# One wait moved on VectorE and two drains taken out of GpSimd's queue, in the expert stage of a three-stage kernel

## The reference

```python
def _moe2_ref(x, w_gate, w1, w2):            # N, D, E, F = 3072, 512, 8, 1024
    logits = x @ w_gate
    expert_idx = np.argmax(logits, axis=1)
    probs = np.exp(logits - logits.max(-1, keepdims=True))
    probs /= probs.sum(-1, keepdims=True) + 1e-09
    gate_w = probs[np.arange(N), expert_idx]
    for e in range(E):
        mask = expert_idx == e
        h = np.maximum(x[mask] @ w1[e], 0.0)
        out[mask] = gate_w[mask, None] * (h @ w2[e])
```

## Time and profile before

| | |
|---|---|
| median of 3 runs | 1037.83 us (1036.77, 1037.83, 1040.45) |
| the profiled execution's own time | 1036.77 us |
| its span | 1035.1 us |
| mean granted TensorE clock | 0.993 |
| busy: PE, DVE, ACT, POOL | 1003.8, 647.5, 583.5, 410.9 us |

### The profile page before, as it was taken

One profiled execution on the slowest core, in us unless ns is written; L12 is line 12 of the kernel. 1 busy time (PEld: TensorE's weight loads), 2 busy tenths in 40 slices (PEclk: granted clock), 3 DMA queues, 4 the chain that ended last, 5 costly groups with the idle time before them and its releaser, 6 DMA issues.

```text
span 1035.1 us, 19854 instructions
## 1 busy us (share of the span) xinstructions
PE 1003.8 (97%) x6222; PEld 819.4 (79%) x6223; DVE 647.5 (63%) x1207; ACT 583.5 (56%) x1255; POOL 410.9 (40%) x397
## 2 busy tenths in 40 slices
PE   8988999999999999999999999997999999999998
PEld 5777778888888888888888778786888888888886
DVE  5876788878867877887688679855223424325221
ACT  7877778766676667667666667624223324225221
POOL 3676444444543454455345357722111111112111
PEclk9999999999999999999999999998999999999999
DMA  8999614700920290064009942117311512411111
GB/s 301 357 403 348 256 41 135 232 1 11 314 84 0 100 307 0 10 234 163 0 18 373 366 149 72 41 42 294 123 41 48 190 42 84 159 41 40 31 48 37
DMA packets 58528, 143.26 MB, mean 138 GB/s; under 512 B 4967, under 2 KB 10727, under 8 KB 58480
## 3 DMA queue, kind: packets, MB, share of 16 engines
q1 hardware_dynamic: 51680, 121.07, 33.0%
q0 software_dynamic: 6800, 21.56, 6.2%
HBM read 71.08 MB, written 72.32 MB: 139 GB/s over the span
## 4 chain that ended last, share of the span: by engine, by line
PE 76%; issue 7%; SPq 5%; ACT 4%; DMA 3%; DVE 3%; POOL 1%; ACTq 0%; DVEq 0%; POOLq 0%
PE PS L511 20%; PE PS L670 19%; PE PS L542 14%; PE PS L551 13%; SPq L463 4%; PE PS L535 2%; ACT prob L819 2%; PE PS L613 2%; PE PS L690 2%; DMA x_raw<-w_exp 1%; PE PS L528 1%; DVE PS L1001 1%; DMA qk<-qk_all 1%; PE PS L583 1%; DMA e_raw<-w_exp 1%
## 5 line engine op out<-in xcount | busy, mean ns | idle before, releaser
L511 PE MATMUL PS<-xs,weights 128*128 (+1 forms) x1152 | 282.7, 394 | 0.0
L511 PEld LDWEIGHTS PS<-xs,weights 128*128 128x128 f32 x1152 | 212.6, 188 | 43.1
L670 PE MATMUL PS<-weights,g_hi 128*128 128x512 f32 x768 | 238.6, 392 | 7.6 <-POOL g_lo L1344 4.6
L1344 POOL TENSOR_TENSOR g_lo<-g_sb,g_hi 128x512 fp32r<-128x512 f32 x96 | 123.9, 1291 | 272.8 <-ACT g_hi L899 272.8
L670 PEld LDWEIGHTS PS<-weights,g_hi 128*128 128x128 f32 x768 | 142.8, 188 | 43.2 <-POOL g_lo L1344 9.1
L670 PE MATMUL PS<-weights,g_lo 128*128 128x512 f32 x384 | 149.6, 390 | 0.0
L542 PE MATMUL PS<-weights,xg_hi 128*128 (+1 forms) x448 | 143.3, 401 | 0.5 <-issue 0.2
L880 ACT ACTIVATE b_ln<-PS,cf 128x512 f32<-128x512 f32 x96 | 65.9, 686 | 132.8 <-PE PS L511 132.8
L551 PE MATMUL PS<-weights,h_hi 128*128 (+1 forms) x432 | 136.1, 396 | 0.1
L1347 POOL TENSOR_TENSOR den<-den,b_r 128x512 f32<-128x512 f32 x96 | 127.7, 1330 | 2.1 <-ACT b_r L907 2.1
L1099 DVE SCALAR_TENSOR_TENSOR den<-den,b_r 128x512 f32<-128x512 f32 x96 | 70.2, 731 | 50.9 <-POOL den L1347 50.9
(11 more groups left out here) (190 smaller groups left out, 1605.0 us busy)
## 6 DMA issues: line engine op xcount, KB each, us to landing
rows_by_expert<-pad_rows SPq DMA_DIRECT2D x40, 1028.0 KB, 15.1
e_raw<-w_exp SPq DMA_DIRECT2D x34, 512.0 KB, 6.7
qk<-qk_all SPq DMA_DIRECT2D x32, 480.0 KB, 6.6
vw<-v_all SPq DMA_DIRECT2D x32, 384.0 KB, 6.0
rows_by_expert<-pad_rows SPq DMA_DIRECT2D x8, 1285.0 KB, 18.2
w_raw<-w_mlp SPq DMA_DIRECT2D x16, 512.0 KB, 8.4
pad_rows<-rows_by_expert POOLq DMA_DIRECT2D x30, 257.0 KB
x_raw<-attention_out_t SPq DMA_DIRECT2D x10, 512.0 KB, 4.5
```

The costliest lines, as they stand in the source:

```text
L511: last = pe.matmul(PS[:, H_BANK + f % 2, :], w[:, wp], rhs, start=k == 0, stop=k == 3 * KT - 1)
L670: last = pe.matmul(PS[:, ACC_BANK + s, :], gp[:, f % 2, s * P:(s + 1) * P], w[:, wp], start=f == 0 and k == 0, stop=f == FT - 1 and k == 2)
L1344: pool.tensor_tensor(g_lo[:, q], g_sb[:], g_hi[:, q].bitcast(F32), ALU.subtract).then_inc(g_lo_done, 1)
```

## The change

Two edits, both in the expert stage. In `finish`, DVE's wait for the second product (`w2e_done`) is moved ahead of the waits for `meta_copied` and `y_done` and so ahead of the copy to `gate_s`. In POOL's program the two drains between `fetch` and what follows are taken out: one ahead of the loop, one in each of its 25 passes.

```diff
             def finish(t):
 
+                dve.wait_ge(w2e_done, upto(w2e_done, t + 1))
                 dve.wait_ge(meta_copied, t + 1)
                 dve.wait_ge(y_done, upto(y_done, t))
                 dve.tensor_copy(gate_s[:], meta_of(t, slice(0, 1))).then_inc(gate_copied, 1)
-                dve.wait_ge(w2e_done, upto(w2e_done, t + 1))
                 dve.wait_ge(gate_copied, t + 1)
                 dve.wait_ge(idx_s_copied, t + 1)
                 dve.tensor_scalar(y_sb[:], PS[:, y_bank(t), :], gate_s[:], None, ALU.mult).then_inc(y_done, 1)
...
             fetch(4, col_of(4))
-            pool.drain()
             tiles = load_sched(pool, R_CNT, 0, NSUB, NSUB + E - 1)
             with pool.Fori(2, tiles) as t:
                 fetch(t + 3, col_of(t + 3))
-                pool.drain()
                 send_y(t)
```

## The result

The changed kernel takes 1045.86 us (median of 6 runs, 1044.07 to 1046.29), the kernel before 1037.74 (6 runs on the same footing, 1036.34 to 1040.85). The ratio, estimated from all of these runs, is 1.0069, 95% interval 1.0051 to 1.0088 (the medians alone, 8.1 us apart, would give 1.0078, inside it): slower by 0.7%, clearly more than can be mistaken for no change, and outside the range I gave. The forecast was 1037.5 and no change.

A forecast was written before the change was run, and what follows sets the result against it. PE's chain of waits was taken to bound the expert stage; drains 0, new experts 0 and moved wait 0.3 us made 1037.1 from the profiled execution, 1038.1 on the median's scale, so 1037.5 was given, range 1035.3 to 1040.7.

The forecast's parts named there:

- In an ordinary tile the drain is worth 0: POOL's loop: removing the drain gains 0, since POOL then waits 2.7 us longer for y_sb and output leaves no sooner.
- Drains 0: Term of the sum: removing POOL's drains, ahead of the loop and in it, changes the time by 0.
- a tail longer by 0.3 us: Sign to check: time from PE's last matmul to the end grows by 0.3 us, from the moved wait.
- about 85 us: POOL's time in drains: one of 8.29 us ahead of the loop, 25 in it with a median of 3.06.
- PE sets the pace: Expert stage: the chain of waits goes from one PE group to the next, 12.30 us a tile.
- The removed drains let the row numbers come 2.7 us sooner: POOL's steady pass: row numbers at about 927.2 instead of 929.91; POOL's wait for y_sb grows by 2.7 us.
- The moved wait: DVE's gate copy now follows PE's last matmul: 0 in the loop, 0.3 us behind the last tile; bounds 0.14 and 0.86.
- The slower rival: POOL copies delay DVE's weight split at three new experts: 4.1 us with the moved wait, 1040.9 us; chance 0.10.
- the rule of the Trainium skill that I quoted: VectorE and GpSimd share an SBUF port lock; a winning GpSimd copy would add 0.6 us over three new experts, 1037.7.
- The small gain at new experts: Rival: PE's 0.36 us loss at each of three new experts goes, 1.1 us, giving 1036.0; chance 0.07.
- the large one at 712 us: Rival: PE's hole from 712 us and the half clock behind it shrink, 8.4 us, giving 1028.7; chance 0.05.
- The hole itself: PE busy 0.66 of 6.02 us from 711.98; another length of this hole before 728 us would show the forecast wrong.

The follow-up runs named there:

- e8: Kernel before, with each loop pass's drain moved from behind the fetch to the head of the pass; 1035.69 us against 1035.10, ratio 0.9997.
- e6: Changed kernel plus a single POOL drain between passes 14 and 15 of the loop; 1038.64 us, ratio 1.0023 to the kernel before.
- e7: Changed kernel plus a single POOL drain between fetch and output of the last pass only; 1039.28 us, ratio 1.0026 to the kernel before.

## Why the prediction was wrong

The step that failed is the price of the removed drains, "In an ordinary tile the drain is worth 0", taken over into the sum as "Drains 0". What I asked there was who waits for the drain, and that answer holds. What I did not ask was what the drain does, and who does it when it is gone. It does 0.082 us of work for each transfer that POOL has issued since the drain before; 26 places off the path gave that work up, and it came back as 6.9 us in the one place with no cover, behind the last landing. The sign that I had named, a tail longer by 0.3 us, came out at 7.3. A row was there to set me asking: POOL's last drain of 129 ns in the epilogue, one transfer behind it. Alone it does not give the price, since it can't tell what is paid once from what is paid per transfer; read as all per transfer, 85 of them make 11 us, by an estimate from above. I had looked at the drains of lines 1391 and 1395 only, and at the tail's chain, whose last piece ends at 1032.74, 2.4 us before the span does. The rest of that stretch I did not account for.

The drains' own sum, "about 85 us", was 91.5, since two of the 25 took over 6 us; nothing hangs on it.

Point by point:

- PE sets the pace, 12.30 us a tile. Right: the same sequence, 129.89 of 130 us busy.
- The removed drains let the row numbers come 2.7 us sooner, and POOL waits so much longer for y_sb. Right. The steady pass of the changed kernel, against the earlier trace rows:

```profile
925.08 0.18 POOL L1318 COPY meta<-pad_rows 128x2 f32 x1 [2.89 <-issue]
926.63 0.56 POOL L1321 DMA_DIRECT2D pad_rows<-rows_by_expert  x1 [1.37 <-PE PS L528]
927.19 0.20 POOL L1373 CAST idx_s<-meta 128x1 uint32 x1
933.46 1.02 POOL L1377 DMA_INDIRECT out<-y_sb,idx_s  x1 [6.06 <-DVE y_sb L1065]
```

  The wait for y_sb grew from 2.92 to 6.06 us, by the 2.7 and the 0.44 of the moved wait.
- The moved wait costs nothing in the loop and 0.3 us in the tail. Right in place, small in size: 0.44. Behind PE's last matmul come two register instructions and an address instruction with gaps of 0.05 us between them, 0.28 us until the copy starts, then 0.19 to the multiply; I had one address instruction and no gaps.
- The slower rival, POOL's copies in the way of the weight split. Wrong in its mechanism, though the sign came true for another reason. In the changed kernel a meta copy and the copy of the row numbers fall into the last split, and the seven chunks take what they took the earlier trace rows:

```profile
937.36 0.81 POOL L1318 COPY meta<-pad_rows 128x2 f32 x1 [2.89 <-issue]
938.92 0.56 POOL L1321 DMA_DIRECT2D pad_rows<-rows_by_expert  x1 [0.75 <-PE PS L528]
939.48 0.96 POOL L1373 CAST idx_s<-meta 128x1 uint32 x1
```

```profile
935.77 8.03 DVE L1156 TENSOR_TENSOR weights<-e_raw,weights 128x1024 f32 x7
943.72 0.68 DVE L1046 TENSOR_TENSOR xg_lo<-PS,xg_hi 128x512 fp32r<-128x512 f32 x1
```

  The POOL copies are stretched again, from 0.2 to 0.8 and 0.96 us, and DVE's chunks are not. The other two splits of the changed kernel agree: 8.03 each, with two POOL copies inside the one at 799.76 (0.99 and 0.97 us) and two inside the one at 873.91 (0.20, not stretched, and 0.95). By the rule of the Trainium skill that I quoted ("SBUF — State Buffer", section "SBUF: two separate sides"), the one that starts first holds the other; in these splits only GpSimd was seen to be held, and the copy that was not held did not hold DVE either.
- The small gain at new experts and the large one at 712 us. Neither came: the first is refuted by the chain of the changed kernel and by e8, the second by the chain's arrival at 727.61. The hole itself has another shape in the changed kernel's trace, which I had named as a sign of being wrong; it is not what failed, as the arrival is the same to 0.02 us.

What stays open is what the 0.082 us are. That they go by the number of transfers and not by bytes or packets is shown; that it is the clearing of some record for each transfer is a guess. Whether other instructions of GpSimd can clear it was not tried.

## What to carry to other kernels

Before a drain, or any wait that nobody seems to need, is priced at its cover, ask what it finishes and who must finish it once it is gone; the place to look is the last uncovered one, the end of the program. In these runs a drain of GpSimd's queue cost 0.05 us and 0.082 us for each transfer issued by it since the drain before. That suggests to put one where that engine waits anyway, often enough that each stays short, and the last of them late but with its cover still to come; in e6 a single one of 5 us in the loop let 0.4 us through, and in e7 one of 7.5 in the last pass let 2.8 through. And account for the whole tail of a profile, from the last matmul to the end of the span, sequencer rows too, since the chain of work stops short of it.

## What I had not expected of the hardware

A drain with a transfer under way waits for its landing (3.06 us in the loop, its issue included; 8.29 ahead of it, with the weight loads running and 35 transfers to work off), and its own work goes on at the same time: in e7 84 transfers took 6.97 us while the fetch landed. The price of a transfer at the drain is the same for an indirect transfer of 128 rows, a plain one of 257 KB and one of 256 bytes: 0.082 us (0.0817 to 0.0825 between neighbours of the table from 2 transfers on, where the shares of the kinds differ; the step from 1 to 2, a single plain one, reads 0.088).
